# Eighteen low halves added and eighteen middle taps moved to an accumulating DMA, in a fused attention and convolution kernel on one core

## The reference

```python
def _moe_ref(x, w_ch1, w_ch2):
    X = np.fft.fft(x, axis=1)
    X = np.fft.fft(X, axis=2)
    mixed = np.real(X).astype(np.float32)
    u = x + mixed
    ...
    un = (u - mu) / np.sqrt(var + 1e-06)
    ch = np.maximum(un @ w_ch1, 0.0) @ w_ch2      # 128 -> 512 -> 128
    return (u + ch).astype(np.float32)

def _moe2_ref(x, w_in, conv_w, w_out):
    h = np.maximum(x @ w_in, 0.0)                 # 128 -> 1024
    hp = np.concatenate([...zeros..., h, ...zeros...], axis=1)
    for k in range(K):                            # K = 3 taps along the tokens
        conv_out += conv_w[k][None, None, :] * hp[:, k:k + S, :]
    gate = 1.0 / (1.0 + np.exp(-conv_out))
    return (h * gate @ w_out).astype(np.float32)  # 1024 -> 128
```

## Time and profile before

| | |
|---|---|
| median of 3 runs | 256.98 us |
| lowest and highest run | 256.5 and 289.55 us |
| the profiled execution, its device time | 256.51 us |
| the profiled execution, its span | 254.7 us |
| TensorE, VectorE, ScalarE, GpSimd busy | 97%, 86%, 62%, 11% of the span |
| granted clock of TensorE | 1.000 over the whole span |

### The profile page before, as it was taken

How to read it: one execution, slowest core, us unless ns; L and a number is a source line. 1 busy time by engine, 2 the same in 40 slices (tenths; PEclk the granted TensorE clock), 3 DMA queues, 4 the chain that set the end, 5 groups by cost and what they waited for, 6 DMA issues and landing times.

```text
span 254.7 us, 4283 instructions
## 1 busy us (share of the span) xinstructions
PE 247.2 (97%) x1522; PEld 210.7 (83%) x1522; DVE 220.2 (86%) x404; ACT 157.0 (62%) x325; POOL 28.4 (11%) x90
## 2 busy tenths in 40 slices
PE   8999999999999999989999999999999999999995
PEld 7999999998989999978887777778778777777752
DVE  0847888899998688897799999999979999997992
ACT  2351733333586547688997766769769576667552
POOL 0000000001603343575200000000000000000000
PEclk9999999999999999999999999999999999999999
DMA  7959730300000000000000000002000002002002
GB/s 249 349 217 348 307 98 0 97 4 0 3 0 1 3 1 0 3 3 3 0 0 3 0 0 0 3 0 89 0 0 3 1 0 87 3 0 87 0 0 88
DMA packets 4340, 13.04 MB, mean 51 GB/s; under 512 B 736, under 2 KB 1504, under 8 KB 4320
## 3 DMA queue, kind: packets, MB, share of 16 engines
q1 hardware_dynamic: 4176, 12.74, 13.7%
q10 hardware_dynamic: 144, 0.03, 0.1%
HBM read 10.54 MB, written 2.23 MB: 50 GB/s over the span
## 4 chain that ended last, share of the span: by engine, by line
PE 46%; DVE 5%; ACT 3%; issue 2%; ACTq 0%
PE ps L600 20%; PE ps L521 7%; PE ps L523 7%; PE ps L522 7%; PE ps L561 5%; DVE arena L1061 2%; DVE arena L1056 1%; ACT arena L722 1%; ACT arena L798 1%; PE ps L552 1%; DVE arena L1068 1%; PE ps L531 0%; DVE x_nat L970 0%; DVE arena L977 0%; DVE x2lo L1004 0%
## 5 line engine op out<-in xcount | busy, mean ns | idle before, releaser
L600 PE MATMUL ps<-arena,wout 128*128 128x364 f32 (+1 forms) x192 | 62.8, 467 | 0.5 <-DVE arena L1068 0.5
L792 ACT ACTIVATE arena<-ps 128x364 f32<-128x364 f32 x96 | 42.6, 482 | 19.0 <-PE ps L523 16.8
L600 PEld LDWEIGHTS ps<-arena,wout 128*128 128x128 f32 x192 | 35.9, 189 | 20.6 <-issue 2.8
L1056 DVE SCALAR_TENSOR_TENSOR arena<-arena,ratio 128x1088 f32<-128x1088 f32 x32 | 43.1, 1346 | 1.9 <-ACT arena L792 1.9
L798 ACT ACTIVATE arena<-arena,base 128x1088 f32<-128x1088 f32 x32 | 38.8, 1211 | 7.3 <-DVE arena L1061 7.1
L1061 DVE SCALAR_TENSOR_TENSOR arena<-arena,ratio 128x1088 f32<-128x1088 f32 x32 | 43.1, 1346 | 0.1
L1068 DVE TENSOR_TENSOR arena<-arena 128x1088 f32<-128x1088 f32 (+2 forms) x36 | 41.3, 1159 | 1.5 <-ACT arena L798 1.3
L521 PE MATMUL ps<-x2hi,wlo 128*128 128x364 f32 x96 | 40.2, 419 | 0.7 <-ACT arena L736 0.4
L523 PE MATMUL ps<-x2hi,whi 128*128 128x364 f32 x96 | 31.5, 328 | 0.0
L522 PE MATMUL ps<-x2lo,whi 128*128 128x364 f32 x96 | 31.5, 328 | 0.0
L843 DVE TENSOR_TENSOR arena<-arena 109x1280 f32<-109x1280 f32 (+1 forms) x12 | 21.9, 1842 | 6.5 <-ACT arena L673 6.4
(11 more groups left out here) (100 smaller groups left out, 404.2 us busy)
## 6 DMA issues: line engine op xcount, KB each, us to landing
arena<-v_d SPq DMA_DIRECT2D x4, 594.0 KB, 3.9
arena<-qT_d SPq DMA_DIRECT2D x3, 545.0 KB, 5.9
arena<-kT_d SPq DMA_DIRECT2D x3, 544.5 KB, 5.0
out_d<-arena SPq DMA_DIRECT2D x3, 544.0 KB, 2.7
cos_t<-cos_d SPq DMA_DIRECT2D x1, 926.5 KB, 5.9
sin_t<-sin_d SPq DMA_DIRECT2D x1, 926.5 KB, 7.7
arena<-qT_d SPq DMA_DIRECT2D x2, 272.5 KB, 3.8
wraw<-w_d SPq DMA_DIRECT2D x2, 256.0 KB, 5.1
```

The lines of the kernel that those rows point to most:

```text
L600: pe.matmul(ps[:, OUT_BANK + t, 0:z - a], wout[:, c, :], gate[:, i % GATES, a:z], start=(c == 0), stop=(c == C2 - 1)).then_inc(wout_done, 1)
L792: act.activation(h2[:, i % HIDDENS, t * TT:(t + 1) * TT], ps[:, bank_p(n), 0:TT], ACT.Relu).then_inc(h2_ready, 1)
L1056: dve.scalar_tensor_tensor(out=gate[:, i % GATES, :], in0=h2[:, i % HIDDENS, 0:S], scalar=ratio[:, 0, i % C2:i % C2 + 1], in1=h2[:, i % HI ...
```

## The change

Four things are changed.

1. `LOW_UNTIL` is 40: `down` is three passes in the last 18 slots too, with 18 more `hidden_low` on VectorE.
2. For the 18 chunks of `ADDED` (2, 4, 6, 8, 9, 10, 12, 14, 15, 16, 18, 20, 21, 22, 24, 25, 26, 28) `left_tap` is gone from VectorE. ScalarE writes `gate = ratio0 * h2[left]` instead (`left_copy`, between the two groups of slots), and GpSimd issues a DMA from `h2[middle]` to `gate` that adds to what is there, 128 rows of 1088 fp32 numbers.
3. `right_tap` of such a chunk waits for that DMA, and stands at the start of VectorE's next iteration.
4. The `h2` buffers are padded so that the DMA's source begins on a 64-byte boundary.

```diff
-LOW_UNTIL = NC1 // 2 + 2
+LOW_UNTIL = NC1
...
+ADDED = tuple(sorted((*range(2, NI - 3, 2), 9, 15, 21, 25)))
+H2_PAD, H2_ROW = 15, 1120
...
-        h2 = room(128, HIDDENS, SP)
+        used[0] += (8 - used[0]) % 16
+        h2 = room(128, HIDDENS, H2_ROW)[:, :, H2_PAD:H2_PAD + SP]
...
+        middle_added = [sem(f"middle_added{n}") for n in range(2)]
...
+        def summed(i):
+            return i - sum(n < i for n in ADDED)
...
+            for n, i in enumerate(ADDED):
+                pool.wait_ge(copied, n + 1)
+                if n >= 2:
+                    pool.wait_ge(middle_added[n % 2], 16 * (n // 2))
+                pool.dma_start(gate[:, i % GATES, :], h2[:, i % HIDDENS, 1:S + 1],
+                               accum_op=ALU.add).then_inc(middle_added[n % 2], 16)
...
+            def left_copy(i):
+                if i == ADDED[0]:
+                    act.wait_ge(ratios_ready, 2)
+                act.wait_ge(h2_ready, NT * (i + 1))
+                if i >= GATES:
+                    act.wait_ge(wout_done, NT * (i - GATES + 1))
+                act.activation(gate[:, i % GATES, :], h2[:, i % HIDDENS, 0:S], ACT.Copy,
+                               scale=ratio[:, 0, i % C2:i % C2 + 1]).then_inc(copied, 1)
...
                     for n in slots_a(i + 1):
                         slot(n)
+                    if i + 1 in ADDED:
+                        left_copy(i + 1)
                     for n in slots_b(i + 1):
...
             def right_tap(i):
-                dve.wait_ge(left_ready, i + 1)
+                if i in ADDED:
+                    n = ADDED.index(i)
+                    dve.wait_ge(middle_added[n % 2], 16 * (n // 2 + 1))
+                else:
+                    dve.wait_ge(left_ready, summed(i) + 1)
...
             for i in range(NI + 2):
-                if i < NI:
+                if i - 1 in ADDED:
+                    right_tap(i - 1)
+                if i < NI and i not in ADDED:
                     left_tap(i)
...
-                if i < NI:
+                if i < NI and i not in ADDED:
                     right_tap(i)
```

More of the change, by code:

```diff
@@ L219, in build @@
         x2hi_ready, x2lo_ready = sem("x2hi_ready"), sem("x2lo_ready")
-        win_done, h2_ready, left_ready, conv_ready, gate_ready, prod_ready, wout_done = (
-            sem(n) for n in ("win_done", "h2_ready", "left_ready", "conv_ready", "gate_ready",
+        win_done, h2_ready, copied, left_ready, conv_ready, gate_ready, prod_ready, wout_done = (
+            sem(n) for n in ("win_done", "h2_ready", "copied", "left_ready", "conv_ready", "gate_ready",
                              "prod_ready", "wout_done"))
         out_ready, tap_step, ratios_ready = sem("out_ready"), sem("tap_step"), sem("ratios_ready")
+        middle_added = [sem(f"middle_added{n}") for n in range(2)]
         stored = sem("stored")
```

## The result

| | before | changed |
|---|---|---|
| median of the runs beside each other (6 and 6) | 256.78 us | 258.94 us |
| the same without the longer executions (4 and 5) | 256.54 us | 258.81 us |
| profiled execution, its span | 256.51, 254.7 us | 258.64, 256.8 us |
| TensorE, VectorE, ScalarE, GpSimd busy | 247.2, 220.2, 157.0, 28.4 us | 245.4, 208.1, 175.3, 42.1 us |

Some executions take some 33 us longer (in the three traces of such, all of it long before layer 2); the ratios, and all medians from here on, leave them out. The ratio is 1.0086, with a 95% interval from 1.0070 to 1.0103: the change makes the kernel 2.2 us slower. That lies inside the wide range (254.0 to 264.5 us) and under 2%, but it is above the 255.5 to 258.5 us of the forecast and a loss that can be measured, where 256.8 us and "no difference that can be measured" were forecast.

A forecast was written before the change was run, and what follows sets the result against it. TensorE's full stream was taken to bound the kernel. Losses of 1.6 (chunk 2), 0.5 (chunks 14 to 16) and 0.2 (end) less 2.2 saved gave +0.1 us; 256.8 us predicted, forecast 255.5 to 258.5, range 254.0 to 264.5.

The forecast's parts named there:

- A down saves 0.15 us: TensorE, 18 downs: three passes take 0.58 us where fp32 took 0.73, saving 2.7 us in all.
- VectorE's relief "at nothing": VectorE: 13.4 us less work over the span, counted as no gain because TensorE does not wait for it.
- Chunk 2: 1.6 us at `up(27)`, by the DMA: Start of layer 2: the DMA delays chunk 2's right tap, then low half 26; TensorE 1.6 us late.
- The 1.0 us for the copy of chunk 2: ScalarE, start of layer 2: the copy ahead of `relu(3)` delays it and `hidden(4)` by 1.0 us.
- Chunks 14 to 16: ScalarE: three copies meet a batch's output and delay a `hidden` with only three banks; 0.5 us taken.
- T = 5 us: Time from the copy's end to the right tap's release by the DMA, bounds 2.7 to 9.4 us.
- The sum: Whole kernel: 1.6 (chunk 2) + 0.5 (chunks 14 to 16) + 0.2 (end) - 2.2 (later downs) = +0.1 us.
- A: Rival: the saving comes through on TensorE, 2.7 us gained, 254.3 us, at best 253.4; chance 0.20.
- B: Rival: a slow adding DMA holds VectorE; 263 us if release takes 8 us, 266 at 9.4; chance 0.19.
- C: Rival: on the shared port each DMA issue waits for VectorE's current instruction, release after 6.3 us, 259.7 us; chance 0.12.
- D: Rival: ScalarE becomes the bound at 92% busy, every copy costs TensorE 0.4 us, 261.3 us; chance 0.07.
- Nowhere else for more than half a microsecond: Sign: TensorE waits for a low half near 134 us, and nowhere else over half a microsecond before the end.

The follow-up runs named there:

- experiment 6: Changed kernel with downs of slots 22 to 25 in fp32 again: 258.13 us, 1.0078; with chunk 2's left tap back on VectorE too: 1.0067.
- experiment 2: Changed kernel without the DMA: right tap waits for the copy alone, middle tap of 18 chunks left out; 258.15 us, 1.0063.
- 5: Changed kernel with chunk 0's left and right taps ahead of low halves 23 and 24 on VectorE: 1.0086.
- experiment 8: Changed kernel without ScalarE's 18 copies; a plain DMA after the relu, left tap of 18 chunks missing: 258.54 us, 1.0070.
- experiment 1: Each half of the changed kernel alone: three-pass downs only, 262.73 us, 1.0241; copies and adding DMAs only, 258.56 us, 1.0086.
- experiment 9: Changed kernel, fewer passes and relieved chunks: slots 22 to 26 fp32, 15 chunks, 256.60 us; passes in last 11 slots, 14 chunks 255.9, five chunks 254.9.
- 7: Changed kernel with an added chunk's right tap behind the next left tap and first low halves on VectorE: 260.77 us, 1.0185.
- late_hole: Changed kernel with fp32 downs in slots 22 to 25 and added chunks' right taps behind the next left tap: 259.54 us, 1.0125.

## Why the prediction was wrong, point by point

- **A down saves 0.15 us.** Right: lateness falls by 0.14 or 0.15 us with each down where nothing waits.
- **VectorE's relief "at nothing", as TensorE does not wait for it.** This is the step that failed. The sum over the span was right (12.1 us less busy, 13.4 forecast), but it says nothing of places. From slot 23 on each `up` waits for the low half before it, in the strict order of an engine that was full. Low halves 22 and 24 cost some 0.7 us each (1.16 in place of 0.42 us of waiting at `hidden(0)`, 0.66 us of lateness up to `hidden(3)`), two terms that the sum did not have. Low half 26 makes `up(27)` 1.3 us late on VectorE's old course, with no DMA ahead of it (experiment 6).
- **Chunk 2: 1.6 us at `up(27)`, by the DMA.** TensorE was to arrive there 0.5 us late and leave 1.6 us late. It arrived 1.43 us late (`hidden(5)`) and left 2.98 us late (`hidden(6)`). Place and releaser came out as forecast, the cause did not, so that is luck: without the DMA the wait is the same 1.44 us (experiment 2). The forecast had the right tap of chunk 2 start when the DMA lets it, at 131.95; it started at 133.19 with no wait, right behind the product of chunk 0, itself 1.7 us later than before (131.99, before 130.26). That comes from VectorE's full course, on which waits for low halves 23 and 24 and ScalarE's copy of chunk 2 lie beside each other; removing either uncovers the other (5, 6, 8).
- **ScalarE.** Busy 18.3 us more, 20 forecast; a copy is 1.21 us. The 1.0 us for the copy of chunk 2 is right as a term: 0.96 us where TensorE comes on time (experiments 1 and 6). In the changed kernel it adds 0.45 us, as low halves 22 and 24 have made TensorE late already. Chunks 14 to 16: 0.5 forecast, 0.7 measured (experiment 8).
- **T = 5 us.** At the end it is 5.3 us from the start of waiting, the copy's end at 231.7, to the right tap at 236.97. T over 4.8 us was to be added in full, and was: 0.5 us in place of 0.2.
- **The sum.** 2.98 us late by `hidden(6)` where 1.6 were forecast: this is 1.4 us of the 2.0 that the sum was short of; 0.2 in the middle and 0.3 at the end are most of the rest.
- **The rivals.** A didn't happen. B is void: landing 4.6 to 5.0 us. C's 259.7 us is the nearest to what was measured, but its mechanism didn't happen: in all 18 the issue took 0.87 us but for one of 1.07, with VectorE's two-input instructions around most of them, and 0.87 us as well at 223.61, where VectorE stood idle from 223.0 to 224.89. By the rule of the Trainium skill (SBUF — State Buffer, "Who interferes with whom") that descriptor writing is not held by them, the trace agrees. D is seen only at the two places named, not along the stream. "Nowhere else for more than half a microsecond" did not hold: 1.16, 0.56 and 0.75 us ahead of `up(27)`.

## What to carry to other kernels

A saving on a full engine that is bought with work on a helper must be priced at each place where the full engine waits for that helper, in the helper's own order; the helper's busy share over the span, even with 13% spare and relief on top, says nothing of it. Where a late instruction is found, look for a second chain of the same length before undoing the first, and begin such a change behind the fill, where the first rows show the helper early. Relief that occupies a third engine has the same price: five relieved chunks beat fourteen (experiment 9).

## What the runs showed of the hardware

The clock granted to TensorE fell to 0.50 (1.2 GHz) late in a wait of 3.15 us, for 6.8 us (experiment 1); 1.2 us after a wait of 1.87 us, for 3.4 us (8); and 0.3 us after a wait of 1.34 us that followed one of 0.19 us, for 3.4 us (7). It stayed at 1.00 over waits of 1.14 to 1.45 us in the other kernels, and over 1.28 and 1.20 us that lay 7.6 us apart (`late_hole`). In experiment 1, 3 us of waiting become a loss of some 6.

A DMA of GpSimd from SBUF to SBUF, 128 rows of 4352 bytes, lands after 2.9 us as a copy and after 4.7 us when it adds; single ones that add took 5.3 to 6.5 us in other kernels of this case, and why is open. The Trainium skill (DMA: Bandwidth & Descriptors, "Anatomy of one DMA — SWDGE (gpsimd) path") gives an estimate of 3.3 us for the copy, near the 2.9 measured; the 1.8 us for adding were shown only here.
